# Row-sum guard moved from VectorE to ScalarE, one reciprocal per head, and the exponential ahead of one eviction

## The reference

```python
def _attn_ref(q, k, v, proj):               # 8 heads, 768 tokens, head size 64, 6 hash bits
    q_bits = (np.einsum('bhsd,dk->bhsk', q, proj) > 0)
    k_bits = (np.einsum('bhsd,dk->bhsk', k, proj) > 0)
    mask = q_bucket[:, :, :, None] == k_bucket[:, :, None, :]   # bucket = bits as a number
    scores = np.where(mask, scale * np.matmul(q, k.transpose(0, 1, 3, 2)), -1e9)
    scores = scores - np.max(scores, axis=-1, keepdims=True)
    attn = np.exp(scores)
    attn = attn / (np.sum(attn, axis=-1, keepdims=True) + 1e-09)
    return np.matmul(attn, v)

x = attn_out.transpose(0, 2, 1, 3).reshape(768, 512)
x = _moe_ref(x, w_gate, w1, w2, capacity)   # 8 experts, argmax of x @ w_gate, relu, 192 slots each
h = x @ w_in                                # 512 -> 2048
return (h * np.tanh(softplus(h))) @ w_out
```

## Time and profile before

| | |
|---|---|
| median of 3 runs | 411.69 us (410.63 to 412.88) |
| the profiled execution | 410.92 us |
| its span, first to last instruction | 409.1 us |
| TensorE busy | 396.4 us (97%), 2667 matmuls |
| weight loads busy | 364.9 us (89%) |
| VectorE busy | 250.4 us (61%), 441 instructions |
| ScalarE busy | 202.0 us (49%), 389 instructions |
| GpSimd busy | 81.5 us (20%), 81 instructions |
| granted TensorE clock | 0.999 |

### The profile page before, as it was taken

How to read it: one execution, slowest core, us unless ns; L and a number is a source line. 1 busy time by engine, 2 the same in 40 slices (tenths; PEclk the granted TensorE clock), 3 DMA queues, 4 the chain that set the end, 5 groups by cost and what they waited for, 6 DMA issues and landing times.

```text
span 409.1 us, 7248 instructions
## 1 busy us (share of the span) xinstructions
PE 396.4 (97%) x2667; PEld 364.9 (89%) x2668; DVE 250.4 (61%) x441; ACT 202.0 (49%) x389; POOL 81.5 (20%) x81
## 2 busy tenths in 40 slices
PE   8899999999999999999999999999999999999995
PEld 3578898898999789899999999999988999899984
DVE  5788889989999451311101111129899998877761
ACT  5968968968879321301101110118577555553541
POOL 0920320320600051473733700000000000000005
PEclk9999999999999999999999999999999999999999
DMA  8765922981700055999999999900000000000003
GB/s 295 243 151 153 242 44 60 311 184 41 244 2 0 2 192 174 413 387 345 320 368 372 364 366 372 322 15 0 2 0 2 1 1 2 0 2 0 0 2 154
DMA packets 15595, 62.85 MB, mean 154 GB/s; under 512 B 2896, under 2 KB 3536, under 8 KB 11344
## 3 DMA queue, kind: packets, MB, share of 16 engines
q1 hardware_dynamic: 14176, 58.51, 42.2%
q0 software_dynamic: 960, 3.15, 2.0%
q10 hardware_dynamic: 432, 0.83, 0.6%
HBM read 49.89 MB, written 3.15 MB: 130 GB/s over the span
## 4 chain that ended last, share of the span: by engine, by line
PE 75%; DVE 10%; DMA 5%; ACT 5%; issue 2%; POOL 2%; SPq 0%; POOLq 0%; DVEq 0%; ACTq 0%
PE ps L805 16%; PE ps L830 14%; PE ps L727 13%; PE ps L745 12%; PE ps L659 5%; PE ps L632 5%; PE ps L545 4%; DVE ptl L1194 3%; DVE nmax L1137 3%; PE ps L615 2%; DMA xg<-rows 2%; DMA kk<-in_first 2%; ACT prob L915 2%; PE ps L508 2%; ACT pth L953 2%
## 5 line engine op out<-in xcount | busy, mean ns | idle before, releaser
L727 PE MATMUL ps<-xs,ring 128*128 x512 | 60.1, 277 | 0.1
L727 PEld LDWEIGHTS ps<-xs,ring 128*128 128x128 f32 x512 | 58.8, 191 | 0.8 <-issue 0.5
L745 PE MATMUL ps<-hs,ring 128*128 128x128 f32 (+1 forms) x512 | 59.2, 276 | 0.0
L745 PEld LDWEIGHTS ps<-hs,ring 128*128 128x128 f32 x512 | 58.5, 192 | 0.0
L1194 DVE TENSOR_TENSOR ptl<-ps,pth 128x384 fp32r<-128x384 f32 x96 | 48.8, 550 | 4.3 <-ACT pth L953 4.3
L953 ACT ACTIVATE pth<-ps 128x384 fp32r<-128x384 f32 x96 | 42.2, 495 | 18.6 <-PE ps L659 17.9
L1137 DVE TENSOR_REDUCE nmax<-ps 128x1 f32<-128x768 f32 x48 | 45.7, 955 | 5.1 <-PE ps L545 4.1
L545 PE MATMUL ps<-ops 128*128 128x384 f32 x192 | 44.1, 351 | 1.8 <-ACT prob L915 1.4
L915 ACT ACTIVATE prob<-ps,nmax 128x768 f32<-128x768 f32 x48 | 43.5, 907 | 1.7 <-DVE nmax L1137 1.6
L659 PE MATMUL ps<-cfs,prob 128*128 128x128 f32 x288 | 41.5, 277 | 1.9 <-DVE ptl L1194 1.8
L805 PE MATMUL ps<-yh,wih 128*128 128x384 f32 x128 | 43.0, 336 | 0.0
(11 more groups left out here) (161 smaller groups left out, 654.1 us busy)
## 6 DMA issues: line engine op xcount, KB each, us to landing
ring<-in_w SPq DMA_DIRECT2D x32, 1024.0 KB, 7.7
winraw<-in_w_in SPq DMA_DIRECT2D x8, 512.0 KB, 8.1
woutraw<-in_w_out SPq DMA_DIRECT2D x8, 512.0 KB
ops<-kh SPq DMA_DIRECT2D x12, 192.0 KB, 3.5
ops<-qh SPq DMA_DIRECT2D x6, 384.0 KB, 5.6
xg<-rows SPq DMA_DIRECT2D x1, 1539.0 KB, 7.1
raw<-in_vt SPq DMA_DIRECT2D x4, 384.0 KB, 5.7
raw<-in_qt SPq DMA_DIRECT2D x3, 384.0 KB, 6.9
```

Source lines behind the costliest of these rows:

```text
L727: last = mm(ps[:, fc // 2, (fc % 2) * WIDE:(fc % 2) * WIDE + W], wa[:, 2 * fc // KF, kd, P * (fc % (KF // 2)):P * (fc % (KF // 2)) + P], x ...
L745: last = mm(ps[:, 4 + half * KD // 2 + k, 0:W], wb[:, half, fc, P * k:P * k + P], hs[:, fc, 0:W], start=(fc == 0), stop=(fc == KF - 1))
```

## The change

In VectorE's loop the guard and the reciprocal after every third unit are gone (16 pairs). ScalarE makes the guarded sums instead, six columns at a time, at the end of every sixth unit: a Relu of `rowsum` with a bias of 1e-9 that comes from a new 128x1 tile, `tiny`, which VectorE fills once at the start. VectorE takes the reciprocal of the six columns in a new helper, `invert_sums`, right ahead of `scale_out` of the same head, and for the last head after the loop. On ScalarE, `prepare("B", n - 1)` moves behind the exponential of unit n + 1, but for n = 3. Only in units 7, 19, 20, 31 and 32 does it contain work there: the eviction of qo. The new tile shifts the tiles behind it by 64 bytes per partition.

```diff
--- before.py
+++ after.py
@@ -131,6 +131,7 @@
         bounds = place("bounds", [P, E + 1, 2], I32)
         mark = place("mark", [P, 4], F32)
         toki = place("toki", [P, NT], U32)
+        tiny = place("tiny", [P, 1], F32)
         sloti = place("sloti", [P, NT], U32)
         rows = nc.dram_tensor("rows", [T, DM + 1], F32, kind="Internal").ap()
 
@@ -217,7 +218,7 @@
 
...
-                  "S", "max", "P", "T", "hi", "lo", "PV", "OT", "xw", "fw", "fr", "pa", "pd", "vs", "rc",
+                  "S", "max", "P", "T", "hi", "lo", "PV", "OT", "xw", "fw", "fr", "pa", "pd", "vs", "rc", "tiny",
                   "zy", "bnd", "Hw", "Ha", "Hd", "Yw", "ya", "yd",
                   "chain", "rc1", "na", "sia", "sid", "soa", "sod", "ph", "sip", "sop", "hw", "hc", "ea", "nd", "hnd", "la", "ra", "n1", "n2", "gd", "gha", "gld", "ow", "oa", "od", "vg"]:
@@ -934,14 +935,17 @@
                     act.wait_ge(s["fw"], m // 2 - 1)
                 av(ots[:, (m // 2) % 2, m % 2, :], ps[:, OB, 0:HALF], ACT.Copy).then_inc(s["OT"], 1)
 
+            act.wait_ge(s["tiny"], 1)
             exp(0)
             for n in range(UNITS):
                 if n >= 2 * HT and n % HT == 0:
                     evict(n // HT - 2)
-                if n:
+                if n == 3:
                     prepare("B", n - 1)
                 if n + 1 < UNITS:
                     exp(n + 1)
+                if n and n != 3:
+                    prepare("B", n - 1)
                 prepare("A", n)
                 if n in HIGH:
                     g, parts = HIGH[n]
@@ -953,6 +957,11 @@
                     av(pth[:, (n // HT) % 2, HT * b:HT * b + HT, n % HT, :],
                        ps[:, TB[b], 0:HALF].rearrange("p (a c) -> p a c", c=P),
                        ACT.Copy).then_inc(s["hi"], 1)
+                if n % NT == NT - 1:
+                    h = n // NT
+                    act.wait_ge(s["P"], n + 1)
+                    av(rinv[:, NT * h:NT * h + NT], rowsum[:, NT * h:NT * h + NT], ACT.Relu,
+                       bias=tiny[:, :]).then_inc(s["rc1"], 1)
             evict(HALVES - 2)
             evict(HALVES - 1)
 
@@ -1090,6 +1099,7 @@
 
             V.memset(still[:, :], 0.0).then_inc(s["still"], 1)
             V.memset(small["lg"][:, :, :], 0.0).then_inc(s["lo"], 2)
+            V.memset(tiny[:, :], 1e-9).then_inc(s["tiny"], 1)
             V.memset(bounds[:, :, :], 0).then_inc(s["PV"], 2)
             V.memset(nmax[:, :], 0.0).then_inc(s["OT"], 1)
             V.memset(sloti[:, :], 0).then_inc(s["fr"], 1)
@@ -1169,6 +1179,13 @@
                 V.tensor_tensor(lg[:, :, :], lg[:, :, :], small["ex"][:, :, :], ALU.add).then_inc(s["gt"], 1)
                 dve.wait_ge(s["gt"], h + 1)
 
+            def invert_sums(h):
+
+                cs = slice(NT * h, NT * h + NT)
+                dve.wait_ge(s["rc1"], h + 1)
+                V.reciprocal(rinv[:, cs], rinv[:, cs]).then_inc(s["rc"], 1)
+                dve.wait_ge(s["rc"], h + 1)
+
             def scale_out(h):
 
                 dve.wait_ge(s["fw"], h + 1)
@@ -1184,6 +1201,7 @@
                 if n:
                     prepare("B", n - 1)
                 if fold_at(n - 1) is not None:
+                    invert_sums(fold_at(n - 1))
                     scale_out(fold_at(n - 1))
                 if n + 2 < UNITS:
                     rowmax(n + 2)
@@ -1194,14 +1212,6 @@
                     V.tensor_tensor(ptl[:, m2, HT * b:HT * b + HT, u, :],
                                     ps[:, TB[b], 0:HALF].rearrange("p (a c) -> p a c", c=P),
                                     pth[:, m2, HT * b:HT * b + HT, u, :], ALU.subtract).then_inc(s["lo"], 1)
-                if n % HT == HT - 1:
-
-                    m = n // HT
-                    cs = slice(HT * m, HT * m + HT)
-                    V.tensor_scalar(rinv[:, cs], rowsum[:, cs], 1e-9, None, ALU.add).then_inc(s["rc1"], 1)
-                    dve.wait_ge(s["rc1"], m + 1)
-                    V.reciprocal(rinv[:, cs], rinv[:, cs]).then_inc(s["rc"], 1)
-                    dve.wait_ge(s["rc"], m + 1)
                 if fold_at(n - 1) is not None:
                     add_logits(fold_at(n - 1))
 
@@ -1210,6 +1220,7 @@
 
             def bc(x):
                 return x.unsqueeze(2).to_broadcast([P, NT, E])
+            invert_sums(H - 1)
             dve.wait_ge(s["fw"], H)
             link(V.tensor_tensor(sm["ex"][:, :, :],
                                  ps[:, XB, 0:NT * W72].rearrange("p (t c) -> p t c", c=W72)[:, :, D:W72],
```

## The result

The changed kernel takes 407.81 us (median of 4 runs, 407.07 to 408.47) against 411.72 for the kernel before beside it: a ratio of 0.9904, 95% interval 0.9880 to 0.9928. It is faster, by 3.9 us where 2.9 were forecast, and lies 0.1 us under the range's lower end. Two more comparisons on other occasions gave 407.95 against 411.60 (0.9914, 0.9886 to 0.9942) and 406.65 against 410.10 (0.9918, 0.9903 to 0.9933), so 3.4 to 3.9 us. The profiled execution took 408.47 us.

What follows compares the result with a forecast made beforehand. TensorE, with holes in the attention stretch, was taken as the bound; 1.71 + 0.80 + 0.40 - 0.1 + 0.1 = 2.9 us off 410.92 gave 408.0, forecast as a 408.8 us median. Own range 408.0 to 409.8; 8 in 10: 407.9 to 411.2.

Steps and rivals of the forecast that it cites:

- What bounds the kernel: Attention stretch, 14 to 142 us: TensorE is the bound, with holes that can be won; everything behind moves along.
- the six holes: TensorE waits at n = 6, 13, 19, 25, 31, 37 behind guard and reciprocal; 1.71 + 0.80 + 0.40 us back.
- The prediction's other figure for the slot: ScalarE's new Relu: by the skill's table its slot would be 0.09 us after the overlap.
- the prediction's 0.66: Step 13 and its two likes: without the Relu, 0.66 us would come back instead of 0.57.
- Part 2: ScalarE's exponential ahead of the qo eviction in steps 7, 19, 20, 31, 32: +0.1 us gain, between 0 and 0.2.
- The reciprocals inside: Seven VectorE reciprocals ahead of scale_out, delaying full steps 10 and 22: -0.1 us together, between 0 and -0.4.
- The sum: Whole kernel: 2.9 us off the profiled execution of 410.92 us, giving 408.0, or 408.8 as a median.
- Rival 1: Full ScalarE steps: a new wait half closes three holes, 0.3 us each; 409.6 to 410.5, say 410.0; chance 0.17.
- rival 3: Closed holes open the next, or scatter and gather after attention vary by as much; 411.2 us; chance 0.07.
- Rival 2: GpSimd's memsets hold the reciprocal at step 34 for 2.7 or 6.0 us: 411.5 or 414.8 us; chance 0.10.

Runs made afterwards that it cites:

- e1: The changed kernel with ScalarE's loop order put back as before, so only the guard and reciprocal change remains: 408.04 us against 411.60 for the kernel before.
- e4: The kernel before with each VectorE guard made a reduction over pairs of sum and 1e-9, at the old places: 409.53 us against 411.60.
- e0: The changed kernel run again without any edit: 407.95 us against 411.60 for the kernel before.

## Why the prediction was right in kind and short in size

**The step that failed** is the size of one term of the sum: "I book +0.1 us, between 0 and 0.2" for the exponential ahead of the eviction, which gave 0.37. With it the loop became 3.39 us shorter where 2.9 were forecast. From the median shown that is 408.3, still inside the range; the half microsecond from there down to 407.81, and so below 407.9, lies in no step of the loop, and its cause stays open.

**What bounds the kernel: right.** Of the loop's 3.39 us, 2.92 lie in the six holes named, and what follows the loop moved along, but for the stretch from L704 to L782, which varied by up to 1.85 us with no regard to the change.

**The six holes: right.** Forecast 3 x 0.57 + 2 x 0.40 + 0.40 = 2.91 us. From the table: 0.41 at step 6, 0.52, 0.51 and 0.65 at 13, 25 and 37, 0.40 and 0.43 at 19 and 31: 2.92. The kind of each was right too: at 13 and 25 what is late next is pth. VectorE and ScalarE after the change, answering to the earlier trace rows:

```profile
46.91 0.95 DVE L1147 TENSOR_REDUCE nmax<-ps 128x1 f32<-128x768 f32 x1
48.19 1.02 DVE L1212 TENSOR_TENSOR ptl<-ps,pth 128x384 fp32r<-128x384 f32 x2 [0.32 <-ACT pth L957]
...
46.20 0.30 ACT L963 ACTIVATE rinv<-rowsum,tiny 128x6 f32<-128x6 f32 x1
46.39 0.50 ACT L936 ACTIVATE ots<-ps 128x384 f32<-128x384 f32 x1
...
47.64 0.89 ACT L957 ACTIVATE pth<-ps 128x384 fp32r<-128x384 f32 x2
```

The row maximum follows at once, ptl waits 0.32 us for pth, and the Relu takes a slot of 46.39 - 46.20 = 0.19 us where 0.15 was taken (bounds 0.10 to 0.25). Its duration of 0.30 lies above the 0.24 of the nearest row; the overlap saved the estimate. The prediction's other figure for the slot, 0.09, is not inside its bounds, as it says, but just under them. The 0.19 us that it estimated for the Relu's duration were those of its slot. By its rows ptl could have started at 48.21 + 0.53 = 48.74, where it wrote 48.77: 0.60 us a step by its own rows, where 0.57 was booked. Step 37 closes by more, 0.65: there the Relu costs nothing, for without it the step takes 1.31 in place of 1.32. And without the Relu step 13 takes 1.27, 0.67 less than before, as the prediction's 0.66 says.

**Part 2: the mis-sized term.** The prediction gave as its reason that "No hole is named after it". Steps 8, 21 and 33 got shorter by 0.37 us in all (0.13, 0.11 and 0.14), and e1, which lacks only the new order, is 0.36 and 0.41 longer than two traces of the changed kernel. The lateness was in the trace: steps 8, 21 and 33 took 1.40 us where 1.27 is undisturbed. I had looked only for steps whose transposes start late. Here they start in time, and their second half waits 0.06 to 0.07 us, and PV starts another 0.05 to 0.08 later than that. A search for holes has to run from one mark to the next over the whole step.

**The reciprocals inside: mis-sized the other way.** -0.1 was booked for steps 10 and 22; steps 10 and 11 take what they took (1.35 and 1.27), 12 and 24 are 0.01 to 0.02 longer, which is all that can be theirs: 0.03 us. The 0.21 us on VectorE fit in its slack.

**The sum.** The loop's 3.39 us against 2.9: 0.27 from the reordering, 0.07 from the reciprocals, the rest spread over steps in hundredths. The median came out half a microsecond lower still, with an interval of 1.0 us to either side that covers 3.4. The low end of the range, 407.9, took in the named bounds, but left no room for what varies between traces outside the loop, 0.77 us at the start and 1.85 from L704 to L782. Chance may not be all of it: in ten of eleven comparisons the medians gained 0.02 to 0.53 us more than the loop did, and the loop of the kernel before was traced only once. No run here settles that.

**The rivals.** Rival 1 is half seen: a new wait for pth stands at 13 and 25, but costs 0.15 us, not 0.3. Of rival 3 the first half, new holes, didn't come; the second, a stretch behind the attention that varies by as much, was seen, but not as an effect of the change. Rival 2 was the right mechanism on the wrong instruction. The Trainium skill, "SBUF — State Buffer", section "Who interferes with whom", lists tensor_scalar but not reciprocal among the operations that can take the port pair shared with GpSimd, and says of reductions that they never contend on this chip. The traces agree: beside GpSimd additions took up to 6.75 us, the reductions of e4 0.15. The reciprocal beside GpSimd's subtraction in the changed kernel:

```profile
42.05 0.18 DVE L1186 RECIPROCAL rinv<-rinv 128x6 f32<-128x6 f32 x1
...
40.88 1.84 POOL L429 TENSOR_TENSOR kl<-raw,kh 128x768 fp32r<-128x768 f32 x1 [17.74 <-ACT kh L902]
```

It runs through at 0.18 inside 40.88 to 42.72, and the one at 72.68 likewise; in e1 one starts at 102.86 inside the memset of yh and takes 0.18 too. The addition at that place takes 0.69, and 6.75 beside the memsets, where I gave rival 2 6.0 us of hold. That its price of 414.8 us in all lies near the 415.93 of the kernel with the addition is luck: it stood for 3.1 us more than before, and beside its own kernel before (409.99) that kernel took 5.9 us more. The price left out the holds beside the subtractions, 0.7 us in each of steps 11 and 23, and the half clock of TensorE, 1.07 us in step 36.

## What to carry to other kernels

A small instruction's cost on a path can be its wait more than its work: look at the longest of a group, not the median, and at what ends when it ends. Choose the operation by whether another engine can hold it: the same guard as a reduction was not held in any of its 32 instances, ten of them inside GpSimd operations, and as an addition in another place it once took 6.75 us, and the loop 9.3 us more than the changed kernel's. Size the holes by start-to-start times over whole steps, halves of a step included, and price two parts of a change together when one sets the time at which the other meets something.

## What the runs showed of the hardware that was not expected

The held VectorE addition did not get in between two GpSimd instructions that follow each other at once: in the kernel with the addition at the new place it waited for both memsets, 6.75 us, although it is recorded as starting at 103.67, just ahead of GpSimd's four small memsets, the first at 103.72. That is one instance in one trace.

Behind the loop, from the slot matmuls L704 to the transposes L782, the same changed kernel took 21.68 us in one trace, 20.63 in the second and 19.99 in the third. The four kernels e0 to e4, run on one chip, took 20.6 to 21.7 us, the six run on two other chips 19.8 to 20.0. In the first trace TensorE waits twice for VectorE's copies of xs, and VectorE 1.19 us for something the profile doesn't name:

```profile
148.76 0.71 PE L728 MATMUL ps<-xs,ring 128*128 x4 [0.28 <-DVE xs L1272]
150.24 1.49 PE L728 MATMUL ps<-xs,ring 128*128 x11 [0.77 <-DVE xs L1272]
...
149.81 0.29 DVE L1272 COPY xs<-ps 128x128 f32<-128x128 f32 x1 [1.19 <-remote]
```

That is a microsecond that comes and goes with the run, a third of what this change gains. Its cause was not tried.
